# Six low parts of w_in through TensorE and VectorE in place of GpSimd, in the first half of a chunked attention with two layers behind it

## The chip, the cores and the metric

The kernel runs on one core of a Trainium2 chip. The metric is the device time of one execution in microseconds (us); three timed runs of the kernel before took 1416.2, 1416.87 and 1418.96 us, median 1416.87. Engines are called by the names of the profile: PE (TensorE), DVE (VectorE), ACT (ScalarE), POOL (GpSimd) and SP (SyncE, which here only starts transfers).

## The reference

```
f = sigmoid(f_logit)                                     # (4, 8, 768, 48), as q, k, v
for t in range(768):
    state = f[t][:, None] * state + outer(k[t], v[t])    # per batch and head, 48 x 48
    y[t]  = q[t] @ state
x = y as (3072, 384)
h = x @ w_in                                             # w_in 384 x 2048
x = (h * sigmoid(1.702 * h)) @ w_out                     # w_out 2048 x 384
p = probs / (probs.sum(-1) + 1e-9)
out = sum over e of p[:, e] * (relu(x @ w1[e]) @ w2[e])  # 4 experts, 384 x 1024 x 384
```

All of it is fp32. The large products are made of three products of rounded operands (fp32r): high by high, high by low and low by high, where the high part of a matrix is its rounded copy and the low part is the matrix minus its high part.

## The kernel before

A batch of 768 places is worked as two halves of 384 places, in three chunks of 128, so there are eight halves. The attention of a half runs over 7 levels (0 to 6): at level L the keys and queries of blocks of 2^L places are multiplied by decays, and PE makes scores between the first and second part of each pair of blocks. Per level and chunk there are four kinds of work: ACT copies the queries into a split form (`q_split`, line 984), DVE multiplies the queries by a decay (the fade, line 1292), PE makes the scores (lines 1559 and 1576, ordinary fp32) into one of a few PSUM banks, and POOL multiplies the keys by a decay (`k_T`, line 720) once PE has read them. The scores are then copied under a mask into `scores_T`, by DVE at levels 0 to 4 (line 1317), by ACT at levels 5 and 6 (line 930). After the levels come, chunk by chunk: `k_rows` (a transpose on PE, a copy on ACT), `y` (PE; DVE adds a diagonal part, line 1326, that POOL makes as `v_diag`, line 765, from `diag`, line 1223), `update` (the state, DVE line 1340) and `x` (a transpose on PE, then ACT line 1009 for the high part and DVE line 1348 for the low part).

The first half has no other half's layer beside it: `alone` runs it by itself ("the half alone"). From then on `both` runs the first layer (x @ w_in, hidden; then w_out) of one half beside the attention of the next, and afterwards the experts' layers run by themselves.

The weights w_in and w_out are prepared once: 12 pieces of w_in (128 x 512) and 16 of w_out (128 x 384). Each is loaded by SP into one of 7 stages (three in `work`, four named `stage`), its high part is made by ACT (line 918), its low part by POOL (line 660) or DVE (line 1365), by the list `low_by`. Thirteen pieces are worked inside the half alone, one behind each of thirteen steps (levels 0 to 5, then steps of the chunks), each engine taking its share at the same place in its own order; the first six are pieces of w_in, and of these POOL makes every low part. SP loads a piece into a used stage only when the low part of the piece seven places earlier is made (line 516), and every engine works strictly in the order written, so a load that waits holds the loads behind it: those of f, q and k for the next half (line 465) among them.

The order of each engine is written out by hand: the order of steps is `all_steps`, and each engine emits its own part of a step. Cross-engine order is by semaphores alone. `bank[3]` holds scores of level 0 (and before that, transposed keys), `bank[7]` the same; behind level 0 neither is written again before the layers begin.

Of the kernel before, what the change touches and what calls it, by code (L numbers as in the profile page):

```python
# [16 lines left out]
F32 = mybir.dt.float32  # L17
F32R = mybir.dt.float32r
I32 = mybir.dt.int32
ALU = mybir.AluOpType  # L20
# [8 lines left out]
def moe_of_attention_kernel(nc: bass.Bass, q, k, v, f_logit, w_in, w_out, probs, w1, w2, out, x2_dram):  # L29
# [4 lines left out]
    E, _, FE = w1.shape  # L34
    PAIRS = H // 2
    HB = S // 2
    CH = HB // P
# [60 lines left out]
    OUT_ALONE = ALONE_PIECES - 6  # L98
    pieces = win_pieces[:6] + wout_pieces[:OUT_ALONE]

    low_by = ["pool"] * 7 + ["dve", "dve", "pool"] * 2
    rows_left = wout_pieces[OUT_ALONE:]
    by_dve = {4: win_pieces[6:7], 5: win_pieces[7:8], 6: win_pieces[8:9], 8: win_pieces[9:10],
              9: win_pieces[10:11] + rows_left[7:8], 10: win_pieces[11:12] + rows_left[8:9]}
# [20 lines left out]
    def at(name, shape, dt=F32):  # L125
        size = 4
        for n in shape[1:]:
            size *= n
        t = nc.alloc_sbuf_tensor_at(name, list(shape), dt, offset=place[0])
        place[0] += (size + 31) // 32 * 32  # L130
        return t
# [19 lines left out]
    ident = at("ident", [P, P])  # L151
    attention_end = place[0]
    win_h = at("win_h", [P, KT * FF], F32R)
    win_l = at("win_l", [P, KT * FF], F32R)
# [19 lines left out]
    stages = [work[:, i * WP:(i + 1) * WP] for i in range(3)]  # L174
# [4 lines left out]
    STAGES = len(stages)  # L179
# [166 lines left out]
    all_steps = [("transpose", "gate"), ("decays", 0)] + [s for slot in plan for s in slot]  # L346
# [10 lines left out]
    with ExitStack() as ctx:  # L357
        bank = [ctx.enter_context(nc.psum_tensor(f"bank{i}", [P, 512], F32)) for i in range(8)]
# [3 lines left out]
        sum_a, sum_x, sum_e, sum_b, sum_c = bank[0:5]  # L362
        c_bank = [sum_a, sum_c, sum_b, sum_e]
        y_bank = bank[5:8]

        def sem(name):
            return ctx.enter_context(nc.semaphore(name))
# [9 lines left out]
        early_scores, early_read, early_split = sem("early_scores"), sem("early_read"), sem("early_split")  # L377
        diag_product, diag_ready, v_diag_ready = sem("diag_product"), sem("diag_ready"), sem("v_diag_ready")
        bands_stored, bands_loaded, band_ready = (sem(n) for n in ("bands_stored", "bands_loaded", "band_ready"))
        pads_zero, pool_built, zeros_ready = sem("pads_zero"), sem("pool_built"), sem("zeros_ready")  # L380
        w_loaded = [sem(f"w_loaded{i}") for i in range(STAGES)]
        w_hi_ready, w_lo = sem("w_hi_ready"), {"pool": sem("w_lo_by_pool"), "dve": sem("w_lo_by_dve")}
        unit_ready = sem("unit_ready")
        read_by = {"act": sem("act_read"), "dve": sem("dve_read")}
# [18 lines left out]
                emit_both(n, (n + 1) // 2, (n + 1) % 2, n + 1)  # L403
            emit_moe(HALVES - 1)

        def weights_beside(emit_step, emit_piece):

            done = 0
            for s in all_steps:
                emit_step(*s, 0, 0, 0)  # L410
                if s in after_step:
                    emit_piece(done)
                    done += 1
            assert done == ALONE_PIECES
# [198 lines left out]
        def _(pool):  # L613
# [177 lines left out]
            def alone(b, a):  # L791
                weights_beside(step, weight_piece)
# [116 lines left out]
        def _(act):  # L909
# [126 lines left out]
            def alone(b, a):  # L1036

                def all_of(s, c, n, a, b):
                    step(s, c, n, a, b)
                    if s == "level" and c == LEVELS - 1:  # L1040
                        step("squares", c, n, a, b)

                weights_beside(all_of, weight_piece)
# [111 lines left out]
        def _(dve):  # L1155
# [199 lines left out]
                    .then_inc(g_ready, 1)  # L1355

            def weight_piece(i):
                if low_by[i] != "dve":
                    return
                which, o, width = pieces[i]  # L1360

                dve.wait_ge(w_hi_ready, i + 1)
                src = stages[i % STAGES][:, 0:width]
                hi, lo = (win_h, win_l) if which == "in" else (wout_h, wout_l)
                dve.tensor_tensor(lo[:, o:o + width], src, hi[:, o:o + width].bitcast(F32), ALU.subtract)\
                    .then_inc(w_lo["dve"], 1)

            def alone(b, a):
                weights_beside(step, weight_piece)

            def both(n, b, a, n1):
                for t in ("q", "k"):
# [115 lines left out]
        def _(pe):  # L1488
# [165 lines left out]
            def layer_out(n, j):  # L1654
# [15 lines left out]
                    last = pe.matmul(dst, wl, gh, start=False, stop=j == FT - 1)  # L1670
                last.then_inc(g_used, 1)

            def alone(b, a):
                for s in all_steps:
                    step(*s, 0, 0, 0)

            def both(n, b, a, n1):
                for slot in range(SLOTS):
# [111 lines left out]
```

## Time and profile before

| | |
|---|---|
| median of three timed runs | 1416.87 us (1416.2 to 1418.96) |
| the profiled execution's own time | 1416.88 us |
| its span in the profile | 1415.2 us |
| PE busy | 1388.5 us, 98% |
| PE weight loads busy | 1314.5 us, 93% |
| DVE busy | 913.9 us, 65% |
| ACT busy | 569.3 us, 40% |
| POOL busy | 637.5 us, 45% |
| chain that ended last | PE 94%, POOL 2%, DVE 1%, ACT 1%, issue 1% |

The span is what the profile covers; the execution's own time is 1.7 us more. Shares are means over the whole span: they hold for the long part behind the first 65 us and say little of the half alone, which has to be read by itself.

### The profile page before, as it was taken

The numbers are of one execution on the slowest core, as the hardware profiler recorded it, in microseconds if no ns is written. First come the engines' busy times: TensorE is split into PE (matmuls) and PEld (weight loads), VectorE is DVE, ScalarE is ACT, GpSimd is POOL, SyncE is SP. The second block draws the span as 40 slices with busy tenths as digits, with TensorE's granted clock in tenths as the row PEclk, the third lists the DMA queues.
The fourth block names the chain that finished last, engine by engine and source line by source line (L and its number), as shares of the span: only waits on it lengthen the run. The fifth ranks groups of instructions, "written<-read, shape, count | busy, mean of one in ns | idle before, by whom it ended". The sixth has DMA issues, their size and how long they took to land.

```text
span 1415.2 us, 20981 instructions
## 1 busy us (share of the span) xinstructions
PE 1388.5 (98%) x8092; PEld 1314.5 (93%) x8092; DVE 913.9 (65%) x1376; ACT 569.3 (40%) x975; POOL 637.5 (45%) x719
## 2 busy tenths in 40 slices
PE   6799999999999999999999999999999999999999
PEld 5799999999999999998999999999999999999998
DVE  7785847566665756447666666666666666666666
ACT  5563534444444445245333233332333334433331
POOL 8776555556574847366312122212212454344430
PEclk9999999999999999999999999999999999999999
DMA  9535243342415160022011010101011112222111
GB/s 156 110 95 76 68 53 85 43 96 33 106 25 114 15 112 16 18 90 75 22 34 35 12 34 23 34 12 34 12 34 56 35 34 65 93 67 68 45 57 45
DMA packets 239796, 79.00 MB, mean 56 GB/s; under 512 B 188752, under 2 KB 238160, under 8 KB 239696
## 3 DMA queue, kind: packets, MB, share of 16 engines
q1 hardware_dynamic: 239696, 77.66, 23.5%
q8 instruction: 64, 1.05, 0.3%
q14 instruction: 36, 0.29, 0.1%
HBM read 67.83 MB, written 9.78 MB: 55 GB/s over the span
## 4 chain that ended last, share of the span: by engine, by line
PE 94%; POOL 2%; DVE 1%; issue 1%; ACT 1%; SPq 0%; DMA 0%; POOLq 0%; DVEq 0%; ACTq 0%
PE bank L1757 9%; PE bank L1755 9%; PE bank L1756 9%; PE bank L1705 8%; PE bank L1706 8%; PE bank L1704 8%; PE bank L1576 7%; PE bank L1668 5%; PE bank L1502 5%; PE bank L1504 5%; PE bank L1503 5%; PE bank L1669 5%; PE bank L1670 5%; PE bank L1608 3%; PE bank L1616 1%; PE bank L1625 1%
## 5 line engine op out<-in xcount | busy, mean ns | idle before, releaser
L1458 DVE SCALAR_TENSOR_TENSOR acc<-bank,p_n,acc 128x384 f32<-128x384 f32 x384 | 234.9, 612 | 68.0 <-PE bank L1757 63.0
L788 POOL TENSOR_TENSOR g_l<-sig,g_h 128x384 fp32r<-128x384 f32 x128 | 172.1, 1345 | 221.0 <-ACT g_h L1026 221.0
L1757 PE MATMUL bank<-w_h,h_l 128*128 128x384 f32 x768 | 257.2, 335 | 0.0
L1755 PE MATMUL bank<-w_h,h_h 128*128 128x384 f32 x768 | 257.0, 335 | 0.0
L1756 PE MATMUL bank<-w_l,h_h 128*128 128x384 f32 x768 | 256.9, 334 | 0.0
L1442 DVE TENSOR_TENSOR bank<-bank,x_copy 128x512 f32<-128x512 f32 x192 | 124.5, 694 | 163.7 <-ACT x_copy L1126 99.9
L1704 PE MATMUL bank<-xs,we_h 128*128 128x512 f32 x528 | 205.5, 389 | 1.1 <-DVE h_l L1448 1.1
L1706 PE MATMUL bank<-xs,we_l 128*128 128x512 f32 x528 | 206.4, 391 | 0.0
L1705 PE MATMUL bank<-xs,we_h 128*128 128x512 f32 x528 | 206.3, 391 | 0.0
L839 POOL TENSOR_TENSOR we_l<-we_raw,we_h 128x384 fp32r<-128x384 f32 x96 | 96.8, 1036 | 218.6 <-ACT we_h L1092 218.6
L1354 DVE TENSOR_TENSOR sig<-bank,sig 128x384 f32<-128x384 f32 x128 | 71.0, 555 | 167.1 <-ACT sig L1019 165.7
L1126 ACT ACTIVATE x_copy<-bank 128x512 f32<-128x512 f32 x144 | 86.2, 598 | 222.4 <-PE bank L1706 222.1
L1448 DVE SCALAR_TENSOR_TENSOR h_l<-bank,h_h 128x512 fp32r<-128x512 f32 x192 | 130.6, 681 | 32.0 <-ACT h_h L1120 32.0
L1120 ACT ACTIVATE h_h<-bank 128x512 fp32r<-128x512 f32 x192 | 114.9, 599 | 79.7 <-DVE bank L1442 79.6
L1755 PEld LDWEIGHTS bank<-w_h,h_h 128*128 128x128 f32 x768 | 144.2, 188 | 1.8
L1756 PEld LDWEIGHTS bank<-w_l,h_h 128*128 128x128 f32 x768 | 144.1, 188 | 1.8
L1757 PEld LDWEIGHTS bank<-w_h,h_l 128*128 128x128 f32 x768 | 144.1, 188 | 0.0
L850 POOL TENSOR_TENSOR w_l<-w_raw,w_h 128x384 fp32r<-128x384 f32 x64 | 63.6, 1015 | 174.3 <-ACT w_h L1100 174.3
L1668 PE MATMUL bank<-g_h,wout_h 128*128 128x384 f32 x384 | 136.6, 356 | 1.9 <-POOL g_l L788 1.9
L1502 PE MATMUL bank<-x_h,win_h 128*128 128x384 f32 x384 | 129.1, 336 | 1.3 <-DVE x_l L1348 1.3
L1504 PE MATMUL bank<-x_h,win_l 128*128 128x384 f32 x384 | 129.0, 336 | 0.0
L1503 PE MATMUL bank<-x_l,win_h 128*128 128x384 f32 x384 | 129.0, 336 | 0.0
(145 smaller groups left out, 2572.1 us busy)
## 6 DMA issues: line engine op xcount, KB each, us to landing
we_raw<-in_moe_w SPq DMA_DIRECT2D x32, 384.0 KB, 4.1
w_raw<-in_moe_w SPq DMA_DIRECT2D x32, 384.0 KB, 3.1
v_sb<-in_v SPq DMA_DIRECT2D x24, 192.0 KB, 3.5
x_dram<-work SPq DMA_DIRECT2D x8, 576.0 KB, 3.1
x_raw<-x_dram SPq DMA_DIRECT2D x12, 384.0 KB, 3.8
f_raw<-in_f_logit SPq DMA_DIRECT2D x56, 72.0 KB, 2.0
q_raw<-in_q SPq DMA_DIRECT2D x56, 72.0 KB, 2.1
k_raw<-in_k SPq DMA_DIRECT2D x56, 72.0 KB, 1.9
```

What stands on the lines that cost most here:

```text
L788: pool.tensor_tensor(g_l[:, j % RING, :], sig[:, j % 2, :], g_h[:, j % RING, :].bitcast(F32), ALU.subtract).then_inc(gl_ready, 1)
L1458: dve.scalar_tensor_tensor(acc[:, pr * TT + i, :], y_bank[y % 3][:, 0:DM], p_n[:, col:col + 1], acc[:, pr * TT + i, :], ALU.mult, ALU.add) ...
L1502: pe.matmul(dst, lh, rh, start=i == 0, stop=False)
L1503: pe.matmul(dst, lh, rl, start=False, stop=False)
L1504: last = pe.matmul(dst, ll, rh, start=False, stop=i == len(lhs) - 1)
L1668: pe.matmul(dst, wh, gh, start=j == 0, stop=False)
L1704: pe.matmul(dst[:, :], lh, rh, start=start, stop=False, skip_group_check=True)
L1705: pe.matmul(dst[:, :], lh, rl, start=False, stop=False, skip_group_check=True)
L1706: return pe.matmul(dst[:, :], ll, rh, start=False, stop=True, skip_group_check=True)
L1755: pe.matmul(dst, hh, wh, start=f == 0, stop=False)
L1756: pe.matmul(dst, hh, wl, start=False, stop=False)
L1757: last = pe.matmul(dst, hl, wh, start=False, stop=f == 1)
```

## The change

The low parts of the first six pieces (all of them pieces of w_in) leave POOL. In their place PE multiplies the piece, as it was loaded, by the identity in ordinary fp32 into a free bank, and DVE subtracts the high part from that bank. PE has this product behind the scores of levels 1 to 6, DVE the subtraction behind its part of the same levels. POOL keeps its keys' fades and the diagonal product. The loads that refill the stages wait for DVE's low parts where they waited for POOL's.

```diff
-    low_by = ["pool"] * 7 + ["dve", "dve", "pool"] * 2
+    THROUGH_PE = 6
+    low_by = ["dve"] * THROUGH_PE + ["pool"] + ["dve", "dve", "pool"] * 2
...
+        piece_bank = [bank[7], bank[3]]
...
+        w_raw_ready = sem("w_raw_ready")
...
-        def weights_beside(emit_step, emit_piece):
+        def weights_beside(emit_step, emit_piece, emit_late=None):
...
                 emit_step(*s, 0, 0, 0)
+                if emit_late and s[0] == "level" and 1 <= s[1] <= THROUGH_PE:
+                    emit_late(s[1] - 1)
...
             def weight_piece(i):
-                if low_by[i] != "dve":
+                if low_by[i] != "dve" or i < THROUGH_PE:
                     return
...
+            def late_piece(i):                      # on DVE
+                _, o, width = pieces[i]
+                dve.wait_ge(w_raw_ready, i + 1)
+                dve.wait_ge(w_hi_ready, i + 1)
+                dve.tensor_tensor(win_l[:, o:o + width], piece_bank[i % 2][:, 0:width],
+                                  win_h[:, o:o + width].bitcast(F32), ALU.subtract).then_inc(w_lo["dve"], 1)
...
+            def late_piece(i):                      # on PE
+                _, o, width = pieces[i]
+                pe.wait_ge(w_loaded[i % STAGES], 16 * (i // STAGES + 1))
+                if i < 2:
+                    pe.wait_ge(early_read, CH)
+                else:
+                    pe.wait_ge(w_lo["dve"], i - 1)
+                pe.matmul(piece_bank[i % 2][:, 0:width], ident[:, :], stages[i % STAGES][:, 0:width],
+                          start=True, stop=True).then_inc(w_raw_ready, 1)
...
             def alone(b, a):
-                for s in all_steps:
-                    step(*s, 0, 0, 0)
+                weights_beside(step, lambda i: None, late_piece)
```

DVE before, from the copies of level 1 to the copies of level 2 (`scores_T` are the scores kept under the mask, `q_T` the queries):

```order
L1317 COPY_PREDICATED scores_T<-early_mask,bank 128x256x2 [waits early_read,early_scores] x3
L1292 TENSOR_TENSOR q_T<-q_T,decays 128x4x16x4 [waits split_ready,decay_ready]
L1292 TENSOR_TENSOR q_T<-q_T,decays 128x4x16x4 [waits split_ready] x2
L1317 COPY_PREDICATED scores_T<-mask,bank 128x128x4 [waits early_read,unit_ready] x3
L1292 TENSOR_TENSOR q_T<-q_T,decays 128x4x8x8 [waits split_ready,decay_ready]
```

DVE now, the same place:

```order
L1324 COPY_PREDICATED scores_T<-early_mask,bank 128x256x2 [waits early_read,early_scores] x3
L1380 TENSOR_TENSOR win_l<-bank,win_h 128x512 [waits w_hi_ready,w_raw_ready]
L1299 TENSOR_TENSOR q_T<-q_T,decays 128x4x16x4 [waits split_ready,decay_ready]
L1299 TENSOR_TENSOR q_T<-q_T,decays 128x4x16x4 [waits split_ready] x2
L1324 COPY_PREDICATED scores_T<-mask,bank 128x128x4 [waits early_read,unit_ready] x3
L1380 TENSOR_TENSOR win_l<-bank,win_h 128x512 [waits w_hi_ready,w_raw_ready]
L1299 TENSOR_TENSOR q_T<-q_T,decays 128x4x8x8 [waits split_ready,decay_ready]
```

A subtraction from a bank stands between the copies of a level and the fades of the next, and waits for PE's product.

POOL before, from the fades of the keys of level 1 to those of level 3:

```order
L720 TENSOR_TENSOR k_T<-k_T,decays 128x4x32x2 [waits early_scores] x2
L660 TENSOR_TENSOR win_l<-work,win_h 128x512 [waits w_hi_ready]
L689 MEMSET state 128x384
L720 TENSOR_TENSOR k_T<-k_T,decays 128x4x16x4 [waits unit_ready,decay_ready,kg_ready]
L720 TENSOR_TENSOR k_T<-k_T,decays 128x4x16x4 [waits unit_ready] x2
L660 TENSOR_TENSOR win_l<-work,win_h 128x512 [waits w_hi_ready]
L696 TENSOR_TENSOR diag_prod<-q_raw,k_raw 128x384 [waits k_loaded2,q_loaded2]
L720 TENSOR_TENSOR k_T<-k_T,decays 128x4x8x8 [waits unit_ready,decay_ready,kg_ready]
```

POOL now, the same place:

```order
L727 TENSOR_TENSOR k_T<-k_T,decays 128x4x32x2 [waits early_scores] x2
L696 MEMSET state 128x384
L727 TENSOR_TENSOR k_T<-k_T,decays 128x4x16x4 [waits unit_ready,decay_ready,kg_ready]
L727 TENSOR_TENSOR k_T<-k_T,decays 128x4x16x4 [waits unit_ready] x2
L703 TENSOR_TENSOR diag_prod<-q_raw,k_raw 128x384 [waits k_loaded2,q_loaded2]
L727 TENSOR_TENSOR k_T<-k_T,decays 128x4x8x8 [waits unit_ready,decay_ready,kg_ready]
```

The subtractions of w_in are gone; the product for the diagonal follows the keys of level 2 at once.

PE before, the scores of levels 1 and 2 and the first of level 3, with the numbers of the banks:

```order
L1559 MATMUL bank4<-q_split_57,k_T_55 128x128 x4
L1559 MATMUL bank5<-q_split_57,k_T_55 128x128 x4
L1559 MATMUL bank6<-q_split_57,k_T_55 128x128 x4
L1576 MATMUL bank0<-q_split_57,k_T_55 128x128 x4
L1576 MATMUL bank1<-q_split_57,k_T_55 128x128 x4
L1576 MATMUL bank2<-q_split_57,k_T_55 128x128 x4
L1576 MATMUL bank0<-q_split_57,k_T_55 128x128 x4
```

PE now, the same place:

```order
L1574 MATMUL bank4<-q_split_57,k_T_55 128x128 x4
L1574 MATMUL bank5<-q_split_57,k_T_55 128x128 x4
L1574 MATMUL bank6<-q_split_57,k_T_55 128x128 x4
L1697 MATMUL bank7<-work_76,ident_67 128x512
L1591 MATMUL bank0<-q_split_57,k_T_55 128x128 x4
L1591 MATMUL bank1<-q_split_57,k_T_55 128x128 x4
L1591 MATMUL bank2<-q_split_57,k_T_55 128x128 x4
L1697 MATMUL bank3<-work_76,ident_67 128x512
L1591 MATMUL bank0<-q_split_57,k_T_55 128x128 x4
```

A product with the identity stands behind the scores of each level; the first two wait for DVE's copies of level 0 (`early_read`), the later ones for the subtraction two pieces earlier (`w_lo`).

## Rows read from the trace of the kernel before

**Rows 1.** Stretches of the span: busy time of each engine, granted PE clock, DMA share
```profile
14.00:28.00 14.00, 8.82 (x74) 8.25 (x72) 13.85 (x16) 8.29 (x19) 14.00 (x17) 1.00 0.84 165
28.00:36.00 8.00, 6.07 (x32) 6.07 (x33) 6.10 (x12) 5.86 (x12) 2.86 (x4) 0.57 0.67 127
...
64.60:70.00 5.40, 5.31 (x21) 5.34 (x22) 5.20 (x4) 1.75 (x4) 2.43 (x4) 0.68 0.49 136
70.00:1415.00 1345.00, 1338.33 (x7759) 1269.68 (x7758) 860.00 (x1307) 530.14 (x894) 583.33 (x636) 1.00 0.21 52
```

**Rows 2.** PE in order of time: start, length, instruction, idle before and its end
```profile
22.15 2.94 PE L1576 MATMUL bank<-q_split,k_T 128*128 128x128 f32 x24 [1.93 <-ACT q_split L984]
...
29.93 8.09 PE L1576 MATMUL bank<-q_split,k_T 128*128 128x128 f32 x48 [4.84 <-DVE scores_T L1317]
...
39.26 2.94 PE L1576 MATMUL bank<-q_split,k_T 128*128 128x128 f32 x24 [1.24 <-DVE scores_T L1317]
...
42.91 1.16 PE L1576 MATMUL bank<-q_split,k_T 128*128 128x128 f32 x8 [0.70 <-ACT scores_T L930]
...
46.24 1.16 PE L1576 MATMUL bank<-q_split,k_T 128*128 128x128 f32 x8 [0.51 <-ACT scores_T L930]
...
48.24 0.63 PE L1588 MATMUL bank<-ident,k_T 128*128 128x128 f32 x4 [0.85 <-POOL k_T L720]
...
64.69 0.41 PE L1502 MATMUL bank<-x_h,win_h 128*128 128x384 f32 x1 [1.26 <-DVE x_l L1348]
```

**Rows 3.** DVE and POOL, single instructions in order of time
```profile
26.30 1.56 POOL L660 TENSOR_TENSOR win_l<-work,win_h 128x512 fp32r<-128x512 f32 x1
...
26.66 1.47 DVE L1292 TENSOR_TENSOR q_T<-q_T,decays 128x256 f32<-128x256 f32 x1
...
27.82 1.18 POOL L696 TENSOR_TENSOR diag_prod<-q_raw,k_raw 128x384 f32<-128x384 f32 x1
...
28.06 1.22 DVE L1292 TENSOR_TENSOR q_T<-q_T,decays 128x256 f32<-128x256 f32 x1
...
36.33 1.49 DVE L1292 TENSOR_TENSOR q_T<-q_T,decays 128x256 f32<-128x256 f32 x1
...
43.77 1.10 DVE L1292 TENSOR_TENSOR q_T<-q_T,decays 128x256 f32<-128x256 f32 x1 [0.31 <-ACT q_split L984]
```

**Rows 4.** Lines by source, length in ns (min/median/max), first and last start
```profile
L1292 DVE TENSOR_TENSOR q_T<-q_T,decays x18: 403/836/1494, 20.8 to 45.4; 128x256 f32<-128x256 f32 x18
...
L660 POOL TENSOR_TENSOR win_l<-work,win_h x3: 1267/1462/1559, 18.9 to 26.3; 128x512 fp32r<-128x512 f32 x3
...
L660 POOL TENSOR_TENSOR win_l<-stage,win_h x3: 1272/1446/1512, 36.0 to 43.1; 128x512 fp32r<-128x512 f32 x3
...
L1442 DVE TENSOR_TENSOR bank<-bank,x_copy x192: 689/690/700, 652.1 to 1396.1; 128x512 f32<-128x512 f32 x192
...
L1704 PE MATMUL bank<-xs,we_h x528: 387/389/504, 649.1 to 1394.7; 128*128 128x512 f32 x176
```

**Rows 5.** ACT in order of time, the gates of the next half
```profile
31.45 1.48 ACT L953 ACTIVATE f_raw<-f_raw 128x1536 f32<-128x1536 f32 x1 [0.63 <-DMA f_raw<-in_f_logit]
```

**Rows 6.** DVE in order of time behind the levels
```profile
45.77 1.77 DVE L1168 STREAM_TRANSPOSE gate_T<-f_raw 128x1536 f32<-128x1536 f32 x1
...
50.63 0.56 DVE L1326 TENSOR_TENSOR y_rows<-bank,v_diag 128x384 f32<-128x384 f32 x1 [2.65 <-PE bank L1608]
...
53.04 0.56 DVE L1365 TENSOR_TENSOR wout_l<-work,wout_h 128x384 fp32r<-128x384 f32 x1 [0.75 <-ACT wout_h L918]
...
62.20 0.56 DVE L1326 TENSOR_TENSOR y_rows<-bank,v_diag 128x384 f32<-128x384 f32 x1 [1.70 <-POOL v_diag L765]
```

**Rows 7.** SP's transfers in order of time: start, time to issue, destination and source
```profile
29.85 1.42 SPq L516 DMA_DIRECT2D work<-in_moe_w_out  x3
31.39 9.09 SPq L465 DMA_DIRECT2D q_raw<-in_q  x16
...
50.09 1.93 SPq L516 DMA_DIRECT2D stage<-in_moe_w_out  x2
```

More of the change, by code:

```diff
@@ L1366, in weight_piece @@
                     .then_inc(w_lo["dve"], 1)
+            def late_piece(i):
[4 more added lines that the diff above has]
+                                  win_h[:, o:o + width].bitcast(F32), ALU.subtract).then_inc(w_lo["dve"], 1)
             def alone(b, a):
-                weights_beside(step, weight_piece)
+                weights_beside(step, weight_piece, late_piece)
             def both(n, b, a, n1):
```

## The prediction

> **What bounds the kernel now.** I read the stretches first [rows 1]. Behind 70 us PE is busy 1338.3 of 1345 us at the full clock: nothing of the change lies there (it adds no instruction after the half alone and takes none away), so that part only shifts. All that can be won or lost lies before 64.69 us, where the first product of the layers starts [rows 2], and in the few us behind it. In the half alone PE is not the bound: from 14 to 28 us DVE is busy 13.85 of 14.00 us and POOL all of it, PE 8.8 [rows 1].
>
> The order of PE in time says who ends its waits [rows 2]: 4.84 us before level 3 end with DVE's copy of the scores, 1.24 before level 5 with the same, at level 6 the waits of 0.5 to 0.7 us end with ACT. The last one, 1.26 us before the first product of the layers, ends with `x_l` on DVE, and three steps before that stands `y_rows` of the last chunk, which waited 1.70 us for POOL's `v_diag` [rows 6]. So the chain runs DVE (levels 1 to 4), ACT (levels 5 and 6), then PE with DVE, then POOL and DVE.
>
> Why DVE is full is in the single instructions [rows 3, 4]. A fade of 128x256 takes 0.40 us at best and 0.84 in the median. The fade that starts at 26.66 takes 1.47 and ends (28.13) just behind POOL's subtraction (26.30 to 27.86); the one at 28.06 ends (29.28) just behind the diagonal product (27.82 to 29.00). DVE stands while POOL works on two SBUF operands.
>
> The Trainium skill says the same ("SBUF — State Buffer", Who interferes with whom): a DVE instruction with two SBUF inputs and a GpSimd one that reads SBUF take turns on one port, and the second waits for the whole of the first; one with at most one SBUF input does not. By that rule alone the new subtraction, which reads a bank, would never wait for POOL; the trace agrees, since 192 subtractions of that shape with one operand in a bank took 689 to 700 ns [rows 4].
>
> There is a clock effect beside it. After the 4.84 us without work PE's granted clock is 0.57 in the mean from 28 to 36 us [rows 1]: mostly the 1.2 GHz level and not 2.4. Levels 3 and 4 together take 8.09 us, 24 records each, while a level at the full clock takes 2.94 [rows 2].
>
> **The change part by part.**
>
> *POOL gives up six subtractions:* six with medians of 1.46 and 1.45 [rows 4], and the shortest 1.27: about 8.5 us. On POOL itself this frees time that is not on the chain before 48 us. What counts is what DVE no longer waits for. From the fades that a subtraction held: at 26.66, 1.47 - 0.40 = 1.07; at 36.33, 1.49 - 0.40 = 1.09; at 43.77, 1.10 - 0.40 = 0.70 [rows 3]. At level 1 the subtraction at 18.9 pushed POOL's three key fades into DVE's three fades; without it they are over before DVE starts, which I put at 1.0, and at level 5 0.45. The last two are my reading, without a row of their own. Sum 4.3 us. Bounds: zero, if POOL's key fades slide into the same places, and 18 x (0.84 - 0.40) = 7.9, all the waiting of the 18 fades by their median [rows 4].
>
> *DVE gets six subtractions* of 128x512 from a bank: 6 x 0.69 = 4.1 us [rows 4].
>
> So on DVE's busy time the two nearly cancel. The gain or loss is decided by where each stands, and I go through the levels.
>
> - Level 1: DVE's copies can start 1.0 earlier; the copies stay as they are; first subtraction -0.6 (back to back). Net +0.4 at the fades of level 2. PE's product for it fits between levels 1 and 2, where PE waits 1.93 us for ACT anyway [rows 2].
> - Level 2: the fade behind POOL's subtraction gives back 1.07, but the diagonal product moves forward by 2 us and now holds the first fade instead of the last. I count +1.0. The scores of level 3 start 1.4 earlier, at 28.5.
> - Level 3: the copies go at PE's pace. PE's second product fills the start of the long gap, which shrinks from 4.84 us to about 2.7. If the clock holds, the chunks come every 0.98 us and not every 1.6. Another 1.3 is won there, but ACT takes most of it back: the sigmoid of the next half's gates waits for its transfer until 31.45 and runs to 32.93 [rows 5], the same as before, and the splits of level 4 stand behind it, 0.86 each. Two more subtractions are paid. At the fades of level 4 I have 34.4 for 36.0: +1.6.
> - Level 4: +1.0 from the fade at 36.33, -0.6 for a subtraction; +2.0 on DVE, +1.9 on PE at level 5 (its product stands in front by 0.4).
> - Levels 5 and 6: ACT's rhythm of splits and copies sets the pace, 1.66 us per chunk (42.91 to 46.24 in two steps [rows 2]). It is passed on unchanged: PE ends level 6 at 45.4 for 47.4, +2.0.
> - Behind level 6 something new is late. PE's sixth product ends about 1 us after the last scores; DVE's sixth subtraction waits for it, and behind it on DVE stand the transpose of the gates (1.77 [rows 6]), `diag` and, through it, POOL's `v_diag`. That transpose started at 45.77 and now starts about 46.6. `v_diag` is ready at 49.7, and the first `y_rows` comes at 49.7 for 50.63: of 2.0 only 0.9 is left there. From the second chunk on the order loosens again, since DVE waited there 0.75 us for ACT's copy of a piece [rows 6] in front of `diag` and no longer does; I get +1.8 at `y_rows` of the last chunk, and 62.9 for 64.69 at the first product of the layers.
>
> *PE gets six products* of 128x512 in ordinary fp32. The trace has none. A 128x128 one is two records, and 24 records take 2.94 us, 0.12 each; by columns that is 2 x 4 x 0.12 = 0.98 us at the full clock and 1.96 at the half one. The lower bound is one rounded pass, 0.39 [rows 4]. I take 0.98. All but the last are covered by PE's waits of 1.93, 4.84, 1.24 and 0.5 us; the last stands in front of `k_rows` and costs about what it lasts minus the 0.85 that PE waits there for POOL's last key fade anyway.
>
> The Trainium skill ("FP8 and Floating Point Precision", TensorE Precision Notes) has true fp32 as four passes. By that page the product would be an estimated 4 x 0.39 = 1.56 us with each pass at its full recorded length; that takes another 0.6 from the gain at the sixth product and nothing elsewhere. No run before shows it.
>
> *SP* loads the third reused stage once DVE has made the third low part, at 34.4 and not at 29.85 [rows 7]. Behind that load stand 16 transfers of q (9.09 us to issue) and 16 of k, then the load at 50.09, which becomes about 55. Its data land about 3 us later, at 58, and ACT wants them near 57 to 58 but has nothing behind them until `x_h` of the last chunk, about 61.6. q and k of the next half are wanted at 62.6 and later. Cost nothing; if SP slips by another 4 us it decides (below).
>
> *The clock*, if it falls all the same: then level 3 stays slow, a product at the half clock (1.96) stands in front of level 4, and I get +0.4 at level 5, +1.4 at level 6 through ACT, and +1.1 at the end.
>
> **Sum.** +1.8 with the clock held, +1.1 without; I take the middle, 1.5. The profiled execution took 1416.88 us (span 1415.2, 1.7 around it), the median of the runs is 1416.87: the same. Forecast 1416.9 - 1.5 = 1415.4 us.
>
> **Rivals.**
>
> *Two clock gains.* From 64.6 to 70 us the granted clock is 0.68 [rows 1]: 5.4 x 0.32 = 1.7 us lost at the very start of the layers, after the thin stretch around 60 to 64. If the shift of 1.8 us puts the first products where that does not happen, the gain is 1.8 + 1.7 = 3.5: 1413.4. For it: the place moves. Against it: the thin stretch before it is as thin as it was, and the clock could as well fall earlier. Chance 0.2.
>
> *The cover was not free (slower).* POOL's key fades and the diagonal product take the place of the subtractions, so that DVE's fades wait as before, and DVE pays 4.1 us for its own; the clock falls at level 3 and the product there costs 0.98 more in front of the copies of level 4; DVE's two waits of 1.0 us at level 3 absorb 1.9. Then +4.1 + 1.0 - 1.9 = 3.2 slower: 1420.1. It decides if less than about 1 of the 4.3 us of relief comes true. Against it: in rows 3 the waits end with a subtraction by name. Chance 0.1.
>
> *Won and given back.* The gain reaches level 6 but the sixth subtraction with the transpose behind it, or the load that slips behind q and k, holds the chunks: `diag`, `v_diag`, `y_rows` keep their old times or `x_h` waits for the stage. 1416.9. For it: only 0.9 is left at the first `y_rows` by my own count. Chance 0.15.
>
> *Forecast* 0.55, own range 1414.4 to 1416.2.
>
> **How the numbers follow.** Range: from the two clock gains with some noise (1412.9) up over no change and run-to-run spread (1417.6); the slower rival is left out. A measurement of this kernel tells no change from one of 0.2%, 2.8 us. Faster by more (below 1414.0): the first rival and a little of the forecast, 0.22. Slower by more: the second, 0.08. Within: 0.70.
>
> **What would show it.** Right: no subtraction of w_in on POOL before 48 us, fades of levels 2 and 4 with at most one long one each, subtractions from the bank at 0.69, PE's gap before level 3 under 3.2 us, first product of the layers at 62.5 to 63.7. The clock in 28 to 36 us tells +1.8 from +1.1. Wrong: fades still at a median of 0.8, DVE waiting for the identity products at levels 2 to 5 (only level 6 may), products far above 1 us at the full clock, or `x_h` of the last chunk waiting for a transfer. Any change of length behind 70 us that is not a shift would be outside all of this.

## The result and the profile after

The changed kernel takes 1420.5 us in the median of nine timed runs (1419.33 to 1424.73), the kernel before beside it 1417.6 (1416.2 to 1419.02): a ratio of 1.003, 95% interval 1.0021 to 1.0038. Here and below the ratio is worked out from the single runs; it is not the quotient of the two medians (here 1.0020). The kernel is slower, and lies outside the range of the prediction. In all the runs told of below one execution, of e14, was in a slower state (1778.05 us at a mean granted clock of 0.73), and it is left out of its median and ratio. The profiled execution took 1419.33 us, its span is 1417.6.

The stretches of the changed kernel, as in [rows 1]:

```profile
14.00:28.00 14.00, 11.91 (x80) 10.60 (x78) 13.62 (x19) 8.33 (x19) 10.37 (x13) 1.00 0.80 162
28.00:36.00 8.00, 4.96 (x31) 4.16 (x32) 6.95 (x13) 5.65 (x11) 2.15 (x3) 0.92 0.53 106
...
55.00:63.00 8.00, 8.00 (x46) 8.00 (x44) 3.43 (x8) 2.21 (x5) 5.33 (x6) 0.57 0.45 142
...
64.60:70.00 5.40, 3.82 (x24) 3.48 (x23) 4.67 (x6) 1.33 (x3) 2.85 (x7) 1.00 0.45 132
```

From 28 to 36 us the granted clock is 0.92 where it was 0.57: level 3 keeps the 2.4 GHz. But now 55 to 63 us has 0.57, where the kernel before had 1.00, and PE is busy in all 8.00 us of it (46 matmul records), where it was busy 6.01 us (51 records) before. PE in order of time, as in [rows 2]:

```profile
28.39 2.94 PE L1591 MATMUL bank<-q_split,k_T 128*128 128x128 f32 x24 [2.49 <-DVE scores_T L1324]
31.18 1.02 PE L1697 MATMUL bank<-work,ident 128*128 128x512 f32 x2
34.84 4.47 PE L1591 MATMUL bank<-q_split,k_T 128*128 128x128 f32 x24 [2.65 <-issue]
39.16 1.02 PE L1697 MATMUL bank<-stage,ident 128*128 128x512 f32 x2
40.02 2.84 PE L1591 MATMUL bank<-q_split,k_T 128*128 128x128 f32 x24
...
46.30 1.16 PE L1591 MATMUL bank<-q_split,k_T 128*128 128x128 f32 x8 [0.51 <-ACT scores_T L937]
47.29 1.02 PE L1697 MATMUL bank<-stage,ident 128*128 128x512 f32 x2
...
67.30 0.41 PE L1517 MATMUL bank<-x_h,win_h 128*128 128x384 f32 x1 [1.26 <-DVE x_l L1355]
```

Level 3 starts at 28.39 for 29.93, level 4 at 34.84 (before, its scores began in the middle of the 8.09 us of both levels), the last scores of level 6 at 46.30 for 46.24, and the first product of the layers at 67.30 for 64.69. DVE behind the levels, as in [rows 6]:

```profile
43.76 0.69 DVE L1380 TENSOR_TENSOR win_l<-bank,win_h 128x512 fp32r<-128x512 f32 x1 [1.42 <-PE bank L1697]
...
48.35 0.69 DVE L1380 TENSOR_TENSOR win_l<-bank,win_h 128x512 fp32r<-128x512 f32 x1 [2.44 <-PE bank L1697]
48.96 1.77 DVE L1175 STREAM_TRANSPOSE gate_T<-f_raw 128x1536 f32<-128x1536 f32 x1
...
52.24 0.56 DVE L1333 TENSOR_TENSOR y_rows<-bank,v_diag 128x384 f32<-128x384 f32 x1 [1.08 <-POOL v_diag L772]
...
64.81 0.56 DVE L1333 TENSOR_TENSOR y_rows<-bank,v_diag 128x384 f32<-128x384 f32 x1 [1.08 <-POOL v_diag L772]
```

The sixth subtraction holds DVE 2.44 us for PE's product; the transpose of the gates comes 3.2 us later than before, and the first `y_rows` now waits for POOL's `v_diag` and no longer for PE. The lines by source, as in [rows 4]:

```profile
L1299 DVE TENSOR_TENSOR q_T<-q_T,decays x18: 410/425/958, 20.3 to 45.5; 128x256 f32<-128x256 f32 x18
...
L1380 DVE TENSOR_TENSOR win_l<-bank,win_h x6: 676/692/727, 26.0 to 48.4; 128x512 fp32r<-128x512 f32 x6
...
L1697 PE MATMUL bank<-stage,ident x6: 592/594/595, 39.2 to 47.7; 128*128 128x512 f32 x6
```

The busy time of the 18 fades alone, in the kernel before and then in the changed kernel:

```profile
20.00:46.20 26.20, 13.52 (x18) 0.87 0.65 97
```

```profile
20.00:46.20 26.20, 9.21 (x18) 0.93 0.59 88
```

The median fade went from 836 to 425 ns and the 18 fades together from 13.52 to 9.21 us, so the relief of 4.3 us was real. DVE's busy time as a whole is 913.0 us for 913.9, although 6 x 0.69 = 4.1 us were added. The sigmoid of the next half's gates, as in [rows 5], and the splits of level 4 behind it:

```profile
32.52 1.48 ACT L960 ACTIVATE f_raw<-f_raw 128x1536 f32<-128x1536 f32 x1 [2.15 <-DMA f_raw<-in_f_logit]
33.91 2.59 ACT L991 ACTIVATE q_split<-q_T 48x256 f32<-48x256 f32 x6
```

The view marks PE's wait before level 4 "issue". But two of the six splits make up one chunk (0.86 us), so the first chunk's are done at about 33.91 + 0.86 = 34.77, and PE starts at 34.84: it waits for the splits, and so for the sigmoid and its transfer.

### The profile page after: what moved, and what is told of

Its sections match the earlier page's. It is cut to its first block, busy times and chain, and to the rows that moved or that the text cites. A ratio compares the mean times of both kernels' runs of the same rounds, so it can differ in the third digit from the quotient of the medians.

```text
span 1417.6 us, 21017 instructions
## 1 busy us (share of the span) xinstructions
PE 1396.7 (99%) x8104; PEld 1319.2 (93%) x8104; DVE 913.0 (64%) x1382; ACT 569.3 (40%) x975; POOL 621.1 (44%) x713
## 3 DMA queue, kind: packets, MB, share of 16 engines
HBM read 67.83 MB, written 9.78 MB: 55 GB/s over the span
## 4 chain that ended last, share of the span: by engine, by line
PE 94%; DVE 2%; POOL 2%; issue 1%; ACT 1%; DMA 0%; SPq 0%; DVEq 0%; POOLq 0%
PE bank L1783 9%; PE bank L1781 9%; PE bank L1782 9%; PE bank L1731 8%; PE bank L1732 8%; PE bank L1730 8%; PE bank L1591 7%; PE bank L1683 5%; PE bank L1684 5%; PE bank L1685 5%; PE bank L1519 4%; PE bank L1518 4%; PE bank L1517 4%; PE bank L1623 3%; PE bank L1631 1%; PE bank L1640 1%
## 5 line engine op out<-in xcount | busy, mean ns | idle before, releaser
L795 POOL TENSOR_TENSOR g_l<-sig,g_h 128x384 fp32r<-128x384 f32 x128 | 165.0, 1290 | 227.9 <-ACT g_h L1033 227.9
L1685 PE MATMUL bank<-g_h,wout_l 128*128 128x384 f32 x384 | 128.6, 335 | 0.0
L1684 PE MATMUL bank<-g_l,wout_h 128*128 128x384 f32 x384 | 128.6, 335 | 0.0
```

Source lines behind the costliest of these rows:

```text
L795: pool.tensor_tensor(g_l[:, j % RING, :], sig[:, j % 2, :], g_h[:, j % RING, :].bitcast(F32), ALU.subtract).then_inc(gl_ready, 1)
L1684: pe.matmul(dst, wh, gl, start=False, stop=False)
```

## The experiments

Four theories. **A**: the sixth subtraction, which waits on DVE for PE's product, holds the transpose of the gates and all behind it. **B**: what moves is mostly where the granted clock falls to 1.2 GHz. **C**: PE's own products cost. **D**: the sigmoid on ACT waits for its transfer and holds the splits of level 4, so that what level 3 wins is lost. All medians, with the kernel before beside them on the same chip. They are not sharp: the half width of an interval, 0.0009, is 1.3 us, and e8 and e16, the same kernel in two rounds of runs, differ by 0.8 us.

| kernel | us | before | ratio, 95% interval |
|---|---|---|---|
| e1_five | 1418.54 | 1417.75 | 1.0001 (0.9992 to 1.001) |
| e2_sixth_late | 1417.95 | 1417.75 | 0.9997 (0.9989 to 1.0006) |
| e3_products_only | 1418.61 | 1417.75 | 1.0002 (0.9993 to 1.0011) |
| e4_from_stage | 1418.62 | 1417.75 | 1.0005 (0.9996 to 1.0014) |
| e5_before_gates_later | 1416.30 | 1417.03 | 0.9996 (0.9988 to 1.0005) |
| e6_sixth_late_gates_later | 1415.89 | 1417.03 | 0.9988 (0.9979 to 0.9997) |
| e7_five_gates_later | 1415.88 | 1417.03 | 0.9989 (0.9981 to 0.9998) |
| e8_after_gates_later | 1417.71 | 1417.03 | 0.9998 (0.9989 to 1.0006) |
| e9_five_gates_later_filled | 1415.85 | 1418.05 | 0.9986 (0.9977 to 0.9995) |
| e10_before_filled | 1416.15 | 1418.05 | 0.9989 (0.998 to 0.9998) |
| e13_after_paired | 1418.22 | 1416.92 | 1.0013 (1.0003 to 1.0022) |
| e14_sixth_late_paired | 1416.42 | 1416.92 | 0.9997 (0.9988 to 1.0006) |
| e15_both_paired | 1415.54 | 1416.92 | 0.9988 (0.9979 to 0.9997) |
| e16_gates_later_paired | 1416.93 | 1416.92 | 1.0 (0.9991 to 1.0008) |

**The sixth piece (A).** e1 leaves it with POOL; e2 keeps it and only moves DVE's subtraction behind the first chunk's `diag`. PE's product stays where it was in e2, behind level 6, though the expectation speaks of both.

```diff
-    THROUGH_PE = 6                                                          # e1
+    THROUGH_PE = 5
...
-                if emit_late and s[0] == "level" and 1 <= s[1] <= THROUGH_PE:   # e2, last_late for DVE alone
+                if emit_late and s[0] == "level" and 1 <= s[1] <= THROUGH_PE - (last_late is not None):
                     emit_late(s[1] - 1)
+                if s == last_late:                                          # ("diagonal", 0)
+                    emit_late(THROUGH_PE - 1)
```

Expected of e1:

> Only five low parts go through PE and DVE; the sixth stays on POOL, as before. Theory A (the sixth subtraction, which waits for PE's product behind level 6, holds the transpose of the gates and with it diag, v_diag and y_rows): the transpose starts near 45.8 instead of 48.96, the first y_rows near 50.5 instead of 52.24, and the median is 1.5 to 3 us under the changed kernel, 1417.5 to 1419. Theory B (the two stretches at the half clock have moved from places where PE is waited for less to level 4 and the second chunk's y): the median stays at 1419.5 to 1421, whatever DVE's order. Theory C (PE's own products, about 1 us each, in front of scores): a sixth of the loss goes, 0.5 us.

Expected of e2:

> All six, but the sixth product and the sixth subtraction stand behind the transpose of the gates and the first diag (step diagonal of chunk 0) instead of behind level 6. Theory A: transpose near 45.8, first y_rows near 50.5 or a little later, the median 1417.5 to 1419. Theory B: 1419.5 to 1421, as the changed kernel. Theory C: as the changed kernel too, since PE's product now stands in front of the first y.

Both come out at the time of before, inside the range that theory A gave. DVE in e2:

```profile
45.75 1.77 DVE L1177 STREAM_TRANSPOSE gate_T<-f_raw 128x1536 f32<-128x1536 f32 x1
...
48.27 0.69 DVE L1382 TENSOR_TENSOR win_l<-bank,win_h 128x512 fp32r<-128x512 f32 x1 [0.31 <-PE bank L1699]
...
50.61 0.56 DVE L1335 TENSOR_TENSOR y_rows<-bank,v_diag 128x384 f32<-128x384 f32 x1 [1.65 <-PE bank L1625]
```

The transpose no longer stands behind the subtraction, and the first `y_rows` waits for PE again. The times alone do not show it here, as the changed kernel was not run beside them; the paired runs below have its price.

**PE's products (C).** e3 is the kernel before with the six identity products, which nobody reads, and loads that also wait for them. e4 is the changed kernel without them, DVE subtracting from the stage in SBUF.

```diff
+                pe.matmul(piece_bank[i % 2][:, 0:width], ident[:, :], stages[i % STAGES][:, 0:width],   # e3, POOL's subtractions stay
+                          start=True, stop=True).then_inc(w_raw_ready, 1)
...
-                dve.wait_ge(w_raw_ready, i + 1)                             # e4
-                dve.tensor_tensor(win_l[:, o:o + width], piece_bank[i % 2][:, 0:width],
+                dve.tensor_tensor(win_l[:, o:o + width], stages[i % STAGES][:, 0:width],
```

Expected of e3:

> The kernel before, POOL making all low parts, with PE's six identity products added and nobody reading them. Theory C (PE's products cost): slower than before by 1.5 to 3 us. Theory B (they hold the clock up in front of level 3 and so move the drops): level 3 at the full clock, the drops elsewhere, the time anywhere from -2 to +3 us and with a wider spread than before. Theory A: within 0.5 us of before, 1417 to 1418, for no order on DVE has changed.

Expected of e4:

> DVE makes the six low parts at the changed kernel's places, but from the stage in SBUF; PE makes no product. Theory A: the sixth subtraction has nothing to wait for, so the transpose starts near 46.5 and the median is 1417 to 1419, though DVE's subtractions may now wait for POOL. Theory B: no product in front of level 3, so the clock falls there as before, the second drop stays near 66 to 69 us, and the time is at or under 1418. Theory C: no product, the median at 1417 or below.

The products alone cost nothing that shows: the ratio of e3 allows 1.0 us less to 1.6 us more, where C gave 1.5 to 3 more. Its trace does not settle it, as the granted clock was at 0.50 from 31 to 35 and from 58 to 69 us there (theory B expected level 3 at the full clock; it took 4.24 us for 2.94). e4 has no product on PE and is not faster either, 1418.62 us where C gave 1417 or less. It also shows what reading a bank buys; its lines by source:

```profile
L1379 DVE TENSOR_TENSOR win_l<-work,win_h x3: 673/683/1067, 25.8 to 34.7; 128x512 fp32r<-128x512 f32 x3
L1379 DVE TENSOR_TENSOR win_l<-stage,win_h x3: 667/686/1103, 38.8 to 44.8; 128x512 fp32r<-128x512 f32 x3
```

From SBUF two of six subtractions are held (1.07 and 1.10 us), from the bank none (0.727 at most). That difference did not show in the time. C falls at the size it was given.

**The sigmoid (D).** One edit, the sigmoid behind level 4 and not behind level 3, on the kernel before (e5), on e2 (e6), on e1 (e7) and on the changed kernel (e8).

```diff
-    for s, follows in ((("next_sigmoid", 0), ("level", 3)), (("next_turn", 0), ("level", LEVELS - 1)),
+    for s, follows in ((("next_sigmoid", 0), ("level", 4)), (("next_turn", 0), ("level", LEVELS - 1)),
```

Expected of e5:

> The kernel before, with the sigmoid of the next half's gates on ACT behind level 4 instead of behind level 3. Theory D (that sigmoid waits for its transfers until 31.4 to 33.5 us in all six traces and holds ACT's splits of level 4, so that whatever is won at level 3 is lost again): in the kernel before, level 3 ends only at 34.8, so little is there to win, 0 to 1 us under before. Theory A alone (only the sixth subtraction matters): no difference to before, within 0.5 us.

Expected of e6:

> The sixth product and subtraction late, and the sigmoid behind level 4. Theory D: level 4 starts on PE at 32.5 to 33.5 instead of 34.8 to 35.8, the gain goes through levels 5 and 6, and the median lies 1.5 to 2.5 us under the kernel before, 1415.3 to 1416.3. Theory A alone: as with the sixth late only, 1417.5 to 1418.5. If the clock (theory B) decides instead, no shift of the median but a wide spread.

Expected of e7:

> Five low parts through PE and DVE, the sixth on POOL, and the sigmoid behind level 4. Theory D: 1.5 to 2.5 us under before, 1415.3 to 1416.3. Theory A alone: as with five only, 1418 to 1418.7.

Expected of e8:

> The changed kernel with the sigmoid behind level 4. Theory D with A: D gives back 1.5 to 2.5, A keeps its 2 to 3: 1418 to 1419. Theory A alone: 1420 to 1421, as the changed kernel.

e6 and e7 are the first kernels faster than before, in the range that D gave; e5, the edit without the change, is not told from it. e8 is a little under the 1418 to 1419 expected. By the medians e6 and e7 are only 0.4 us under e5 (1416.30 - 1415.89 and 1416.30 - 1415.88), so more than half of what they win over the kernel before is not shown to be the change's. PE and then ACT in e6:

```profile
32.32 2.94 PE L1593 MATMUL bank<-q_split,k_T 128*128 128x128 f32 x24 [0.25 <-DVE scores_T L1326]
...
62.10 0.66 PE L1519 MATMUL bank<-x_h,win_h 128*128 128x384 f32 x1 [1.26 <-DVE x_l L1357]
```

```profile
33.72 1.47 ACT L962 ACTIVATE f_raw<-f_raw 128x1536 f32<-128x1536 f32 x1
```

Level 4 starts at 32.32, with 0.25 us of waiting, where the changed kernel started it at 34.84. The sigmoid runs at 33.72 without a wait: the transfer lands before it. With the sigmoid behind level 3, the fourth level began between 34.3 and 35.8 us in e1, e2, the changed kernel and its repetitions, whenever level 3 had started (28.3 to 29.1). The clock bears on it too: in the seven traces of these kernels (the changed one, e1, e2, e11 to e14) it fell during level 3 or 4 in five, and in the six with the later sigmoid (e6 to e9, e15, e16) in one, e15.

**The clock (B), and repetitions.** e9 and e10 give PE four small products on the identity in each of two idle places (behind the last chunk's `update` and its `x`), on e7 and on the kernel before. e11 and e12 are the changed kernel again, one execution each.

```diff
+            def keep_warm(s, c):
+                if (s, c) in (("update", CH - 1), ("x", CH - 1)):
+                    for _ in range(4):
+                        pe.matmul(bank[7][:, 0:P], ident[:, :], ident[:, :], start=True, stop=True)
```

Expected of e9:

> Five low parts through PE and DVE, the sigmoid behind level 4, and in PE's two waits of the last chunk (1.32 and 1.26 us) four fp32 products of the identity with itself each, about 0.95 us, that nobody reads. Theory B for the second drop (PE's thin work from 58 to 63 us lets the clock fall as the layers begin, where PE is the bound): the granted clock stays up in 61 to 69 us, level 2 of the next half starts 1 to 2 us sooner behind the first product of the layers, and the median is 1 to 2 us under the same kernel without the filling, 1414 to 1415. If the fill does not hold the clock or PE's products delay the transposes: 1415.9 to 1417.

Expected of e10:

> The kernel before with the same filling in the last chunk alone. Theory B: 1 to 1.7 us under before (its clock was at the lower level from 65.9 to 69.3 us), 1415.7 to 1416.7. Else within 0.5 us of before or a little slower.

Expected of e11 and e12:

> The changed kernel once more, for a second trace. Theory A: the transpose of the gates about 0.6 us behind the sixth product again, the first y_rows at 51.5 to 52.5. Theory B: the stretches at the lower clock lie elsewhere than in the first trace (34.6 to 38 and 55.6 to 62), and the time differs by what they cover: near 1424 if a chunk's y is covered and the start of the layers too, near 1419.5 if only one is.

> The changed kernel a third time. The same as for the second.

The same stretch in e6 and then in e9:

```profile
61.00:66.00 5.00, 3.90 (x15) 3.93 (x16) 4.22 (x5) 1.08 (x3) 1.26 (x5) 0.66 0.38 104
```

```profile
61.00:66.00 5.00, 4.30 (x27) 3.82 (x26) 4.73 (x6) 1.50 (x4) 2.34 (x6) 1.00 0.41 114
```

Filled, the granted clock stays at 1.00, and neither trace shows a fall behind 60 us. Even the kernel before, filled, becomes faster (0.9989). But two traces are few: of the 16 unfilled ones four (the changed kernel, e11, e13, e16) have no fall at the start of the layers either. And the trace of e10 does not show the gain where it was looked for. From the first product of the layers to its end it took 1416.60 - 62.53 = 1354.1 us, the kernel before with its fall 1416.88 - 64.69 = 1352.2; 1.4 us of the difference are PE's waits marked "issue" (1.6 us in seven, for 0.2 in one). That the fill is faster because it holds the clock is therefore not shown. e9 missed the 1414 to 1415 us expected for it, e10 came in its range, and e9 is only 0.3 us under e10.

The repetitions differ by more than the change. Theory A expected the first `y_rows` at 51.5 to 52.5 us; it came at 50.70 and 54.16, each time 5.94 us behind the last scores. e11 took 1415.73 us, with the granted clock at 1.00 from 28 us on, e12 1421.59. PE in e11, then DVE in e11:

```profile
34.38 2.92 PE L1591 MATMUL bank<-q_split,k_T 128*128 128x128 f32 x24 [1.44 <-DVE scores_T L1324]
...
44.76 1.16 PE L1591 MATMUL bank<-q_split,k_T 128*128 128x128 f32 x8 [0.50 <-ACT scores_T L937]
...
64.00 0.41 PE L1517 MATMUL bank<-x_h,win_h 128*128 128x384 f32 x1 [1.26 <-DVE x_l L1355]
```

```profile
46.81 0.69 DVE L1380 TENSOR_TENSOR win_l<-bank,win_h 128x512 fp32r<-128x512 f32 x1 [2.43 <-PE bank L1697]
47.42 1.77 DVE L1175 STREAM_TRANSPOSE gate_T<-f_raw 128x1536 f32<-128x1536 f32 x1
...
50.70 0.56 DVE L1333 TENSOR_TENSOR y_rows<-bank,v_diag 128x384 f32<-128x384 f32 x1 [1.08 <-POOL v_diag L772]
...
61.51 0.56 DVE L1333 TENSOR_TENSOR y_rows<-bank,v_diag 128x384 f32<-128x384 f32 x1 [1.07 <-POOL v_diag L772]
```

And ACT in e12, then PE in e12:

```profile
33.40 1.48 ACT L960 ACTIVATE f_raw<-f_raw 128x1536 f32<-128x1536 f32 x1 [3.14 <-DMA f_raw<-in_f_logit]
```

```profile
35.73 5.46 PE L1591 MATMUL bank<-q_split,k_T 128*128 128x128 f32 x24 [3.62 <-issue]
```

In e12 the transfer of f landed at 33.4, level 4 came 1.35 us later than in e11 and, behind a gap of 3.62 us, at the lower level of the clock (5.46 us for 2.92). Its first product of the layers is at 67.46 us, 3.5 behind that of e11. The other 2.4 us of the difference lie behind it, where the clock of e12 was low once more, from 69 to 72 us.

**Both repairs on one chip.** e13 is the changed kernel, e14 is e2, e15 is e6, e16 is e8.

Expected of e13:

> The changed kernel, both causes in. If the causes add up: 2.5 to 3.5 us over before on the same chip. If the clock adds its own: over 4, or under 2.

Expected of e14:

> The sixth product and subtraction late, the sigmoid where it was. If the causes add up: 1.5 to 2.2 us under the changed kernel on this chip, about before plus 1. If the sixth is the whole of the loss: 2.5 to 3 under it, at before.

Expected of e15:

> The sixth late and the sigmoid behind level 4. If the causes add up: 3.7 to 4.3 us under the changed kernel, 1 to 1.5 under before.

Expected of e16:

> The sixth where the change has it, the sigmoid behind level 4. If the causes add up: 2 to 2.7 us under the changed kernel and 1.5 to 2 over the kernel with both.

Against e13 the late subtraction gives 1418.22 - 1416.42 = 1.8 us (and 1416.93 - 1415.54 = 1.4 with the later sigmoid in), the later sigmoid 1418.22 - 1416.93 = 1.3 (and 1416.42 - 1415.54 = 0.9 with the late subtraction in), both together 1418.22 - 1415.54 = 2.7. That fits two separate causes, but with medians as loose as these it does not prove that they add up. Most of the sizes expected were missed: e13 lies 1.3 us over the kernel before and not 2.5 to 3.5 (under 2 was named as a sign that the clock adds its own), e14 0.5 under it and not 1 over, e15 2.7 under e13 and not 3.7 to 4.3, e16 1.3 under e13 and not 2 to 2.7, and 1.4 over e15 for 1.5 to 2. With both repaired the change is 1.4 us under the kernel before; e5, the sigmoid alone on the kernel before, is 0.7 under it. The largest distance is that of e9, 1418.05 - 1415.85 = 2.2 us below the kernel before beside it.

## Why the prediction was wrong

The span up to the layers can be taken apart by three marks. From the start of the last scores of level 6 to the first `y_rows`, and from there to the first product of the layers:

| trace | last scores | to first y_rows | to the layers | first product | whole execution |
|---|---|---|---|---|---|
| predicted (46.24 - 2.0) | 44.24 | 5.46 | 13.2 | 62.9 | 1415.4 |
| before [rows 2, 6] | 46.24 | 4.39 | 14.06 | 64.69 | 1416.88 |
| e10, before filled | 44.09 | 4.39 | 14.05 | 62.53 | 1416.60 |
| the changed kernel | 46.30 | 5.94 | 15.06 | 67.30 | 1419.33 |
| e11, the same | 44.76 | 5.94 | 13.30 | 64.00 | 1415.73 |
| e2, subtraction late | 46.22 | 4.39 | 14.05 | 64.66 | 1416.77 |
| e6, sigmoid later too | 43.65 | 4.40 | 14.05 | 62.10 | 1415.89 |

Of the 67.30 - 62.9 = 4.4 us by which the trace missed the forecast, 2.06 lie in the levels, 0.48 in the step to `y_rows` and 1.86 in the chunks. Beside e11, the same kernel with the clock at its full level, the 4.4 us part in another way: 67.30 - 64.00 = 3.3 us came with the clock, which fell at level 4 (1.54, a landing 0.47 us later included) and in the chunks (1.76), and 64.00 - 62.9 = 1.1 us to the order of the work. Two steps of the prediction failed, then: the sigmoid that was to be where it had been, and the clock, for which the sum allowed 0.7 us (+1.8 or +1.1) and only for level 3.

*The relief of DVE against its own work* (4.3 and 4.1 us): right, as the fades show. Level 3 was forecast at 28.5 and came at 28.39, with a gap of 2.49 us ("under 3.2") and the full clock.

*"the sigmoid of the next half's gates waits for its transfer until 31.45 and runs to 32.93, the same as before"*: this step failed. It was read as a fixed time, but the landing is not one: 32.52 in the changed kernel, 32.05 in e11, 33.40 in e12, 33.51 in e2. Nor is it chance alone. In all eight traces where DVE makes these low parts and the sigmoid waits it starts at 31.95 us or later (e1), and in the kernels where POOL makes them at 31.45 or earlier (before, e3, e10). SP took 10.06 to 11.76 us to issue the 16 transfers of f in the kernels with the change and 9.78 to 10.64 in the others. Why is open. The fades of level 4 came at 34.85, not 34.4, and in e11 the last scores 0.5 us late (44.76 for 44.24). The larger error is what stood next: with the sigmoid in ACT's order ahead of level 4's splits, PE's start of level 4 is set by that transfer, so the win of level 3 turned into an idle stretch between levels 3 and 4 (2.65 us), and there the clock fell. It did so in e12 and e14 too, with 3.62 and 2.76 us idle there; in e11 and e1, with 1.44 and 2.12, it did not. I had treated the clock as an affair of the gap before level 3 alone ("If the clock holds"). The later sigmoid, which removes the wait, is worth 1.3 and 0.9 us in the paired runs.

*"Behind level 6 something new is late"*: the right mechanism, its size a little low. The transpose was to come 46.6 - 44.24 = 2.4 us behind the start of the last scores, and came 2.66 behind it in e11 and in the changed kernel. The row "to first y_rows" has +1.55 where I had 5.46 - 4.39 = +1.07.

*"From the second chunk on the order loosens again"*: right by the rows, 0.75 us are given back (13.30 for 14.05), as I had read from DVE's wait of 0.75 for ACT. So A costs 1.55 - 0.75 = 0.8 us in the traces, but 1.8 and 1.4 in the paired medians and 1417.71 - 1415.89 = 1.8 between e8 and e6. The other 0.6 to 1.0 us is not placed; the medians of e8 and e16, one kernel, differ by as much (0.8).

*PE's product*: 1.02 us where I took 0.98, in two records of 0.594 us. PE is free again sooner, as records overlap: the next instruction starts 40.02 - 39.16 = 0.86 us behind the product's start. Rounded products of the same shape follow each other by 0.23 us, though each record has 0.39:

```profile
649.09 0.39 PE L1704 MATMUL bank<-xs,we_h 128*128 128x512 f32 x1
649.32 0.40 PE L1705 MATMUL bank<-xs,we_h 128*128 128x512 f32 x1
```

The Trainium skill ("FP8 and Floating Point Precision", TensorE Precision Notes) counts four passes for true fp32, and the trace agrees within 7% if passes are counted from start to start (0.86 against 4 x 0.23 = 0.92). What was wrong is the estimate of 1.56 us in the prediction, which added up four whole records.

*The subtraction from a bank*: 0.69, held by nobody (0.727 at most). The Trainium skill ("SBUF — State Buffer", Who interferes with whom) has it that a DVE instruction with at most one input in SBUF does not wait for GpSimd, and one with two inputs there takes turns with GpSimd's reads; the trace agrees with the first, and the two held subtractions of e4 fit the second.

*SP's slip*: harmless. The last load that I was unsure of went out at 54.07 (I had about 55), and no engine waited for its data:

```profile
54.07 1.24 SPq L523 DMA_DIRECT2D stage<-in_moe_w_out  x2
```

*The clock behind the chunks*: I gave it one direction, a rival in which the fall at 64.6 us goes away. It did go away (0.68 to 1.00), and another stood in the `y` of the chunks (0.57 from 55 to 63 us, 15.06 - 13.30 = 1.8 us). That rival ought to have had a counterpart: a fall that is moved can land on fuller work.

*The sum.* A forecast of -1.5 met +2.9 by the medians of the nine runs (+3.0 to +5.4 by the interval) and +1.3 in e13. From 29 us on both e11 and e10 run at the full clock, and the first product of the layers comes 64.00 - 62.53 = 1.5 us later in e11: up to there the order of the changed kernel loses, 0.7 in the levels (most of it the sigmoid, at 32.05 for 31.37) and 0.8 behind them. As long as ACT's sigmoid set level 4, the relief did not get past it. But the first product does not settle the whole time, and the prediction took it to ("that part only shifts"). From it to the end the executions took 1351.3 us (e16) to 1355.2 (e7), a spread of 3.9 us and as wide as all that is argued about here. So e11 as a whole was 0.9 us shorter than e10, and e6, whose first product is 2.6 us ahead of that of the kernel before, ended 1.0 ahead. Two things are seen behind the first product: the fall of the clock at the start of the layers, and the waits of PE marked "issue", 0.23 us each, seven of them in e10 and one in the kernel before. What remains between +1.3 and +2.9 goes with the executions: the changed kernel spreads over 1415.7 to 1424.7 us, the kernel before stayed within 1415.2 to 1419.9. Why the nine runs held more long executions than those of e13 stays open.

*The rivals.* "Won and given back" came nearest: the sixth subtraction did take the place of the wait removed, though the gain had been lost at level 4 already. "The cover was not free" gave about the measured size by a cause that the fades exclude: the size is luck.

## What to carry to other kernels

When an engine on the chain is relieved, look first at what is next in the strict order of the other engines, and treat an instruction that waits for a transfer as a gate whose time changes from one execution to the next, not as a fixed mark: here moving one sigmoid behind one level was worth 1.3 and 0.9 us, where the whole change was meant to bring 1.5. A new wait that is put ahead of the head of another chain (the transpose of the gates) can cost what it lasts there; two instructions later the same subtraction left the marks of the kernel before as they were (4.39 and 14.05 us in e2). Where an idle stretch is moved, ask which work will be running at the lower clock behind it, and compare traces of one kernel with each other before two kernels are compared. A companion edit that helps, such as the later sigmoid, belongs on the kernel before as well, or its gain is put down to the change.

## What the hardware showed unexpectedly

- The 16 transfers of f take 11.29 us to issue on SP (9.8 to 11.8 over all traces). The sigmoid that waits for their last data started at 32.05 to 33.40 us in four executions of the changed kernel (with e11 to e13), and at 31.45 in the kernel before.
- The stretch at 1.2 GHz lay at 28 to 35 and 66 to 69 us before, at 35 to 38 and 55 to 62 in the changed kernel, from 34 to 41 and from 69 to 72 in e12, from 29 to 33 in e13 and nowhere in e11; the last three are the changed kernel again. e11 and e12 differ by 5.9 us (1421.59 - 1415.73), the transfer included.
- With eight small products in idle places the granted clock was 1.00 behind 60 us in both traces taken, and the kernel before went from 1418.05 to 1416.15 us. That the one caused the other is not shown.
- In the part behind 70 us PE has a wait of 0.23 us marked "issue" ahead of a `y` of a chunk, once in six traces (before: 0.2 us), two or three times in seven and five to seven times in e4, e7, e9, e10 and e12 (e10: 1.6 us); its cause was not looked for.
